# Running product: partial products summed in PSUM by TensorE, normalisation in four-step pieces

## The reference

```
mag = sqrt(a_re^2 + a_im^2);  scale = min(mag, 0.999) / (mag + 1e-6)
a_n = a * scale                                  # complex, per token and dimension
S_re, S_im = a_re_n*S_re - a_im_n*S_im + k (x) v, a_re_n*S_im + a_im_n*S_re
y[t] = q[t] . S_re
```

## Time and profile before

| | us |
|---|---|
| median of 3 runs | 813.38 (813.21 to 814.14) |
| profiled execution, its own time | 813.1 |
| its span | 811.3 |
| PE busy in the span | 674.3 (83%) |
| DVE busy | 655.7 (81%) |
| ACT busy | 480.1 (59%) |

### The profile page before, as it was taken

One profiled execution on the slowest core, in us unless ns is written; L12 is line 12 of the kernel. 1 busy time (PEld: TensorE's weight loads), 2 busy tenths in 40 slices (PEclk: granted clock), 3 DMA queues, 4 the chain that ended last, 5 costly groups with the idle time before them and its releaser, 6 DMA issues.

```text
span 811.3 us, 17899 instructions
## 1 busy us (share of the span) xinstructions
PE 674.3 (83%) x6792; PEld 630.3 (78%) x6792; DVE 655.7 (81%) x1241; ACT 480.1 (59%) x673; POOL 213.5 (26%) x183
## 2 busy tenths in 40 slices
PE   0634342089999999938999999999999999999997
PEld 0413231088888888928999999999999989999997
DVE  7998999989999999966868667756898687676572
ACT  7688898567766666453656555545644544554541
POOL 3200000011111111013343456632344332233422
PEclk9765655589999999969999999999999999999999
DMA  7221311018833333455765665667665755665640
GB/s 190 60 71 44 88 44 29 0 51 146 173 118 107 116 95 109 138 105 192 246 226 181 222 207 192 223 197 243 209 200 186 257 187 197 223 225 188 233 151 30
DMA packets 78342, 123.77 MB, mean 153 GB/s; under 512 B 12986, under 2 KB 60582, under 8 KB 78096
## 3 DMA queue, kind: packets, MB, share of 16 engines
q1 hardware_dynamic: 71120, 106.43, 43.2%
q0 software_dynamic: 7168, 16.64, 5.8%
HBM read 111.30 MB, written 13.75 MB: 154 GB/s over the span
## 4 chain that ended last, share of the span: by engine, by line
PE 46%; DVE 6%; DMA 2%; issue 1%; ACT 1%; POOL 0%; POOLq 0%; SPq 0%; DVEq 0%
PE banks L1281 20%; PE banks L1345 14%; PE banks L1328 8%; PE banks L1256 2%; DVE w_lo L899 2%; PE banks L1266 1%; DMA raw<-w1b 1%; DMA raw<-w1a 1%; DVE mix_spot L1544 1%; DVE mix_hT_lo L1643 1%; PE banks L1263 1%; DVE w_lo L905 1%; ACT w_hi L889 0%; DMA xbuf<-mix_y,to_scatter 0%; DVE mix_y L1667 0%
## 5 line engine op out<-in xcount | busy, mean ns | idle before, releaser
L1281 PE MATMUL banks<-mix_xT_hi,w_hi 128*128 128x240 f32 x576 | 159.8, 277 | 0.6 <-DVE mix_xT_lo L1652 0.6
L1281 PE MATMUL banks<-mix_xT_lo,w_hi 128*128 128x240 f32 x576 | 159.2, 276 | 0.0
L1281 PE MATMUL banks<-mix_xT_hi,w_lo 128*128 128x240 f32 x576 | 158.0, 274 | 0.0
L709 PE MATMUL banks<-sq,ident 128*128 128x288 f32 x104 | 49.7, 662 | 81.4 <-ACT sq L626 81.4
L1382 ACT ACTIVATE mix_hT_hi<-banks 128x480 fp32r<-128x480 f32 x96 | 54.8, 572 | 105.6 <-PE banks L1281 103.2
L1281 PEld LDWEIGHTS banks<-mix_xT_hi,w_hi 128*128 128x128 f32 x576 | 108.9, 189 | 0.9 <-issue 0.8
L1281 PEld LDWEIGHTS banks<-mix_xT_hi,w_lo 128*128 128x128 f32 x576 | 109.4, 190 | 0.0
L1281 PEld LDWEIGHTS banks<-mix_xT_lo,w_hi 128*128 128x128 f32 x576 | 109.2, 190 | 0.0
L709 PEld LDWEIGHTS banks<-sq,ident 128*128 128x128 f32 x104 | 32.7, 325 | 97.2 <-ACT sq L626 62.8
L1643 DVE SCALAR_TENSOR_TENSOR mix_hT_lo<-banks,mix_hT_hi 128x480 fp32r<-128x480 f32 x96 | 62.7, 653 | 55.7 <-ACT mix_hT_hi L1382 53.6
L1345 PE MATMUL banks<-w_hi,mix_hT_hi 128*128 128x384 f32 (+1 forms) x256 | 89.8, 351 | 1.5 <-DVE mix_hT_lo L1643 1.5
(11 more groups left out here) (236 smaller groups left out, 1696.9 us busy)
## 6 DMA issues: line engine op xcount, KB each, us to landing
raw<-w1b SPq DMA_DIRECT2D x16, 1536.0 KB, 7.8
raw<-w2b SPq DMA_DIRECT2D x16, 1536.0 KB, 6.7
raw<-w1a SPq DMA_DIRECT2D x8, 1536.0 KB
raw<-w2a SPq DMA_DIRECT2D x8, 1536.0 KB, 7.8
ring<-a SPq DMA_DIRECT2D x9, 864.0 KB, 4.9
qk<-q SPq DMA_DIRECT2D x48, 96.0 KB, 2.3
qk<-k SPq DMA_DIRECT2D x48, 96.0 KB, 2.3
vt<-v SPq DMA_DIRECT2D x24, 192.0 KB, 2.5
```

What stands on the lines that cost most here:

```text
L709: last = pe.matmul(banks[:, c, 0:STEP * PSEG].rearrange("p (t s) -> p t s", t=STEP), ident[:, :], sq[:, c * STEP:(c + 1) * STEP, j, :], st ...
L1281: last = pe.matmul(pU[g % TURNS][:, n * N:(n + 1) * N], w1p[m][:, b, c, f * P:(f + 1) * P], xT[s][:, c, 0:N], start=(c == 0 and (s, m) == ...
```

## The change

The sum of a step's partial products moves from VectorE to TensorE, and the running product lives in PSUM. `prod` for a half holds four blocks of 36: P_re*a_re, P_re*a_im, P_im*a_re, P_im*a_im. Three matmuls with a 128x128 identity, or with a negated identity, add them into a slot of 72 columns of a PSUM bank: 72 columns (start of the sum), 36 and 36. VectorE's next product reads the slot directly. Six steps (`BLOCK`) fill a bank; each half has a bank of its own and a second one in turn, so four banks are used. ScalarE copies out blocks of six steps (`spread_out(b)`), both planes and both halves in one copy of 864 elements.

The negated plane and all negations go; the ring has two planes and five groups, and its slot is free once its last product is formed. The squares' sums use banks 4 to 7 for odd and even groups, in matmuls of 216 columns that TensorE issues one at a time between the steps' matmuls (`squares_at`), three groups ahead. The normalisation's four instructions work on four steps each (288 and 576 elements), twelve instructions for a group of twelve steps, and VectorE issues one after most steps and two after a group's last (`parts_at`).

```diff
-    STEP, SPAN, RING = 4, 12, 4
+    STEP, SPAN, RING, BLOCK = 4, 12, 5, 6
...
+        def place_of(t):
+            return t // BLOCK % 2 * 2, t % BLOCK * SLOT
...
                 if g >= RING:
-                    sp.wait_ge(spread, g - RING + 1)
                     for c in range(2):
-                        sp.wait_ge(added[c], starts[g - RING + 1])
+                        sp.wait_ge(multiplied[c], starts[g - RING + 1] - 1)
...
+            def add(t, c):
+                first, col = place_of(t)
+                into = bank[first + c][:, col:col + SLOT]
...
+                if t % BLOCK == 0 and t >= 2 * BLOCK:
+                    pe.wait_ge(spread, t // BLOCK - 1)
+                pe.wait_ge(multiplied[c], t)
+                pe.matmul(into.rearrange("p (j s) -> p j s", j=2), ident[:, :], prod[:, c, RE], start=True, stop=False,
+                          skip_group_check=True)
+                pe.matmul(into[:, IM * HS:(IM + 1) * HS], ident[:, :], prod[:, c, IM, RE], start=False, stop=False,
+                          skip_group_check=True)
+                pe.matmul(into[:, RE * HS:(RE + 1) * HS], negated[:, :], prod[:, c, IM, IM], start=False, stop=True,
+                          skip_group_check=True).then_inc(added[c], 1)
...
+            def squares_at(g, n):
+                if g == 1:
+                    return {3: (3, (0, 1, 2)), 4: (3, (3, 4, 5)), 5: (3, (6, 7)), 6: (4, (0, 1)), 7: (4, (2, 3))}.get(n)
+                if g == 2 and n < 2:
+                    return 4, (2 * n + 4, 2 * n + 5)
+                if n >= 4 and g + 3 < GROUPS and n - 4 < count_of(g + 3):
+                    return g + 3, (n - 4,)
...
+            for t in range(T):
+                g = group_of[t]
+                if t == starts[4]:
+                    embed_turned()
+                for c in range(2):
+                    add(t, c)
+                piece = squares_at(g, t - starts[g])
+                if piece:
+                    sum_squares(*piece)
...
             def step(t):
-                if t == starts[group_of[t]] or t == 1:
-                    dve.wait_ge(negated, group_of[t] + 1)
+                if t == 1 or t % STEP == 0:
+                    dve.wait_ge(scaled, t // STEP + 1)
+                first, col = place_of(t - 1)
+                g = group_of[t]
                 for c in range(2):
-                    if t > 1:
-                        dve.wait_ge(added[c], t - 1)
-                    dve.tensor_tensor(prod[:, c], here(t - 1, IM, 2, c).unsqueeze(2).to_broadcast([P, 2, 2, HS]),
-                                      crossed(t, c), ALU.mult).then_inc(multiplied[c], 1)
-                for c in range(2):
-                    dve.wait_ge(multiplied[c], t)
-                    dve.tensor_tensor(here(t, IM, 2, c), prod[:, c, 0], prod[:, c, 1], ALU.add).then_inc(added[c], 1)
+                    dve.wait_ge(added[c], t)
+                    dve.tensor_tensor(prod[:, c],
+                                      bank[first + c][:, col:col + SLOT].rearrange("p (i s) -> p i s", i=2
+                                                                                  ).unsqueeze(2).to_broadcast([P, 2, 2, HS]),
+                                      ring[:, g % RING, t - starts[g], :, c * HS:(c + 1) * HS
+                                           ].unsqueeze(1).to_broadcast([P, 2, 2, HS]), ALU.mult).then_inc(multiplied[c], 1)
...
+            def parts_at(g, n):
+                if g == 0 or g + 1 == GROUPS:
+                    return 0
+                if g == 1:
+                    return 2 if n >= 2 else 0
+                if g == 2:
+                    return (0, 0, 0, 1, 1, 1, 1, 1, 1, 2, 2, 2)[n]
+                return (0, 1, 1, 1, 1, 1, 1, 1, 1, 1, 1, 2)[n]
```

More of the change, by code:

```diff
@@ L497, in running_products @@
     GROUPS = len(sizes)
-    assert sum(sizes) == T and all(s % STEP == 0 for s in sizes)
+    BLOCKS = -(-T // BLOCK)
+    assert sum(sizes) == T and all(s % STEP == 0 for s in sizes) and starts[2] == 2 * BLOCK and SPAN == 2 * BLOCK
     EARLY = 3
     group_of = [g for g, s in enumerate(sizes) for _ in range(s)]
-    IM, RE, NEG = 0, 1, 2
+    RE, IM = 0, 1
     HS = PSEG // 2
+    SLOT = 2 * HS
+    EMB = BLOCK * PSEG
+    ROUTE = EMB + KC * E
     with ExitStack() as ctx:
@@ L645, in inverses, with spread_out @@
                 act.activation(flat(recip, g), flat(recip, g), ACT.Exp, scale=-1.0).then_inc(exped, 1)
[L647 to L652, removed]
-                for c in range(2):
[L654 to L662, removed]
-                    for c in range(2):
[L664 to L668, removed]
+            def spread_out(b):
+                low, high = b * BLOCK, min(b * BLOCK + BLOCK, T)
+                first, _ = place_of(low)
+                for c in range(2):
+                    act.wait_ge(added[c], high)
+                if high < T:
+                    for c in range(2):
+                        act.wait_ge(multiplied[c], high)
+                else:
+                    act.wait_ge(ended, 2)
+                act.copy(A[:, :, 0:PSEG, low:high].rearrange("p j (c s) t -> p j c s t", c=2),
+                         banks[:, first:first + 2, 0:(high - low) * SLOT].rearrange(
+                             "p c (t j s) -> p j c s t", j=2, s=HS)).then_inc(spread, 1)
             act.preload_act_table_set("sqrt_and_others")
@@ L691, in _ @@
                     act.preload_act_table_set("natural_log_exp_and_others")
[L692 to L694 removed]
                     inverses(g + 2)
[L696 to L698 removed]
+                spread_out(2 * g - 2)
+            spread_out(BLOCKS - 1)
         @block.tensor
         def _(pe):
[L702 to L722 removed]
@@ new lines, in sum_squares @@
+            def sum_squares(g, pieces):
+                first = 4 + g % 2 * 2
+                for n in pieces:
+                    if n == 0:
+                        pe.wait_ge(squared, g + 1)
+                        pe.wait_ge(rooted, g - 1)
+                        if g == 9:
+                            pe.wait_ge(emb_copied, 1)
+                    low, j = n // 2 * (BLOCK // 2), n % 2
+                    high = min(low + BLOCK // 2, sizes[g])
+                    last = pe.matmul(bank[first + low // BLOCK][:, low % BLOCK * PSEG:(low % BLOCK + high - low) * PSEG],
+                                     ident[:, :], sq[:, g % 2, low:high, j, :], start=(j == 0), stop=(j == 1))
+                    if n == count_of(g) - 1:
+                        last.then_inc(summed, 1)
@@ L738, in clip @@
[L738 to L747 removed]
+            refined_at = {-1: 0}
@@ L808, in _ @@
             scale(0)
[L809 to L823 removed]
+            for t in range(1, starts[1]):
+                step(t)
```

209 lines of the change are left out of this document (125 added, 84 removed).

## The result

The changed kernel takes 1043.01 us (median of 4 runs, 1042.10 to 1044.16) against 813.76 us (813.21 to 814.57): a ratio of 1.2817, with a 95% interval of 1.2795 to 1.2839. The prediction was 800.3 us, in a range of 791 to 861. It had the wrong sign and the time is outside the range.

A forecast was written before the change was run, and what follows sets the result against it. VectorE was taken to bound the kernel's first stage, to about 163 us. The stage's sums end at 148.5 instead of 161.5 us, plus 0.2 for a longer end: -12.8 from 813.1 gives 800.3 us, range 791 to 861.

The forecast's parts named there:

- a step now needs six matmuls: TensorE, running product: six matmuls with 128x128 weights a step, 0.66 us at the full clock, 1.28 at the half.
- the clock rises in the second group and stays: TensorE's granted clock in the running product's stage goes to full in group two and remains; chance 0.50, 800.3 us.
- Rival A: Running product's stage: the half clock stays and TensorE binds, 18.5 us a group, 858.7 us in all; chance 0.36.
- the queue never empties, so it will rise: TensorE at the half clock: 1.28 us of work against a loop of 1.25 keeps it busy, so the clock rises.
- the rest of the forecast: Running product's stage with six matmuls a step at the full clock: it ends at 148.5 us against 161.5.
- the eight groups to step 120: Running product's stage at the full clock: a group of 12 steps takes 12.3 us in place of 13.5.
- the loop: Round trip of a half's step between VectorE and TensorE: 0.91 us at the full clock, 1.25 at the half.
- the three matmuls: TensorE's part of a half's round trip: 0.52 us at the full clock, 0.86 at the half.
- the last one, from which the forecast took 0.06 off: Last matmul of a half's three on TensorE: 36 columns instead of 113 make it 0.06 us shorter.
- the end of the stage and its handing over: Last product's copy out of PSUM ahead of ScalarE's last copy: 0.2 us longer.
- The product from PSUM: VectorE's product reading the PSUM slot: nothing extra charged, at worst 0.06 us a step, 8 us in all.
- rival C: Running product's stage: matmuls do not wait for weights, the loop is 0.65 us, VectorE binds, 786 us; chance 0.04.

The follow-up runs named there:

- experiment 2: The changed kernel with the running product's matmul calls widened by zeros to 108 and 116 columns, same sums: 884.31 us, ratio 1.0896.
- experiment 7: The changed kernel with fp32r products, squares and identities (one record a call), calls widened up to 292 columns, GpSimd's fill later: 825.35 us, ratio 1.0155.
- experiment 3: The changed kernel with the step's products and both identities in fp32r, one record a call, squares left at fp32: 886.41 us in a single execution.
- experiment 1: The kernel before with series of extra matmuls of 36 to 128 columns queued on TensorE after its last squares; whole time not compared.
- experiment 5: The changed kernel with GpSimd's fill of A's gap starting at step 24 instead of step 12: 1042.08 us.
- experiment 6: The changed kernel widened to 108 and 116 columns, with only the first of three matmul calls per half (four records a step): 819.11 us, ratio 1.0069.
- experiment 8: The kernel before with the clip of the normalisation factor moved from VectorE to GpSimd from group 3 on: 824.85 us, ratio 1.0147.

## Why the prediction was wrong, step by step

**The step that failed first was "a step now needs six matmuls".** It needs twelve. The trace of before had it: the burst of squares is x12 in the earlier trace rows, and the code issues six calls for a group there. I read the burst's length and not its count, and so took a squares' call for one record too. Its price is settled by experiments 2 and 7, both at the full clock: from twelve records to six (with the squares from two to one, and without the fill's 5 us) is 884.3 to 825.4, 59 us. At the half clock the same term weighs more: after against experiment 3 is 1043.0 to 886.4, 157 us, of which 4.6 are the fill's, and 127 steps x 6 x 0.213 is 162.

**The second is "the clock rises in the second group and stays".** Rival A had this right, with a chance of 0.36. The argument "the queue never empties, so it will rise" is refuted by experiment 1: 36 columns back to back stayed at 0.50. The doubt in rival A's own words, that the array streams columns for little of the time, was the right one. Its price is after against experiment 2: 159 us. Put right in the count of records alone, rival A's own sum comes out near: 858.7 + 127 x 1.28 + 70 x 0.36 = 1046.5, against 1043.0, in which 4.6 us are the fill's and not in that sum.

**The third is the rest of the forecast**, and experiment 7 shows it, since it has six records and the full clock: 827.9 in its profiled execution (2.6 above its median) against 800.3. Its last sum ends at 168.4 us instead of 148.5. Of these 19.9 us, 4.8 lie before step 12: 1.7 of them are a later first product, behind the making of the fp32r identities and the clearing of `prod`, and 1.3 are VectorE's instructions for the embeddings between steps 11 and 12, which the kernel before has there too and the forecast left out. Another 3.4 lie in the next group, which starts with a wait of TensorE for ScalarE's first copy out of PSUM and has the clock at 0.50 from 36.3 to 39.7 us; 10.4 in the eight groups to step 120 (13.6 each for 12.3), and 1.4 at the end.

```profile
35.77 0.40 PE L731 MATMUL banks<-prod,ident_r 128*128 128x292 f32 x1 [2.53 <-ACT A L678]
```

In the loop, VectorE follows TensorE after 0.04 us as forecast. TensorE follows VectorE after 0.05 us in 24 of the 33 cases from 51 to 160 us in which it stood idle, and after 0.15 in 9 (106.10 to 106.25 in experiment 7's rows). The 0.12 us that the loop is longer than forecast lie in the three matmuls, which take 0.64 us and not 0.52. About 0.07 of it is the last one, from which the forecast took 0.06 off because it moves only 36 columns. It takes 0.28 us with 256 columns (106.58 in experiment 7's rows), and the changed kernel, in its stretch at the full clock, takes 0.39 for two records 0.11 apart, so 0.28 with 36 columns as well:

```profile
37.44 0.39 PE L727 MATMUL banks<-prod,negated_ident 128*128 128x36 f32 x2
```

From the start of the last matmul to the start of the product it is 0.32 us in both. The rest is the first matmul of 292 columns (0.24 to the next one's start, 0.20 in the row that the forecast used).

The other 7.7 us lie behind the stage. The same ten microseconds in before and in experiment 7 (before has entered the attention stage 7 us earlier, so they are not the same work):

```profile
180.00:190.00 10.00, 10.00 (x188) 9.06 (x191) 9.71 (x13) 5.59 (x13) 2.55 (x2) 1.00 0.61 121
```

```profile
180.00:190.00 10.00, 10.00 (x109) 8.78 (x108) 5.04 (x6) 2.50 (x7) 1.19 (x1) 0.50 0.01 2
```

where DMA moves 121 and 2 GB/s too. In before the clock is at 0.50 for the first 4 us of the attention stage, in experiment 7 from 176.3 to 189.9 us. I had charged 0.2 us for the end of the stage and its handing over; which part the clock has in the 7.7 us was not tested.

**What held.** The product from PSUM takes 306 ns against 298 from SBUF: nothing extra. The pitch of a matmul behind a 128x128 weight load is 0.213 and 0.11 us down to 36 columns, so rival C (columns set the pace) is out. Pieces lie in VectorE's wait and are hidden. ScalarE's copy from PSUM takes 0.88 us for 864 elements, and in the changed kernel no wait of TensorE is put down to it. It is not always in time, though: at step 12 TensorE waits 1.0 us for it in experiment 5 and 2.5 us in experiment 7 (where VectorE's embeddings cover all but about 0.8). The later stages are 3 us longer in the changed kernel.

**What is not settled.** The series of experiment 1 have no pauses, and what pauses between such matmuls do was not measured by itself. The clock's fall at 126 us in experiment 6 comes 4 us after the squares end; why it falls was not tested by itself. Nor was a version with the same sums in fewer fp32 calls.

## What to carry to other kernels

Count records, not calls: divide the count of a line in the profile by the calls in the code before multiplying anything with a pitch. A matmul record in fp32 or fp32r with a full stationary matrix cost 0.11 or 0.21 us here even when it moved only 36 columns, so an identity matmul is a dear adder for 36 columns, and a chain of them that waits for VectorE had to beat VectorE's two sums, 0.29 us a step. And when TensorE's clock is part of a forecast, look for a row whose matmuls move as few columns as yours; in these runs a full queue was no evidence for it.

## What the runs showed of the hardware that was not expected

- The clock does not follow TensorE's busy share alone. With every stretch of experiment 1 busy throughout, it was 0.50 in the series of 36 columns, rose in those of 96 and 128, and kept in those of 72 the level that it had. The changed kernel stayed at 0.50 for 340 us of full work.
- fp32 calls are two records with two weight loads; fp32r and bf16 calls are one. In bf16, 120 matmuls of 36 columns took 3.16 us, 0.026 us each, weight loads included, against 0.112 in fp32 at the same clock. The Trainium skill (TensorE: Matmul & The Clock Gate, Weight-path perf modes) says that fast weight loads apply to 128 weights whose type is not fp32. The bf16 row agrees; the fp32r records, 0.11 us apart, do not show a faster load.
- VectorE slows down beside GpSimd, and by how much depends on the instruction: a TENSOR_SCALAR of 384 elements took 4.99 us beside a fill (0.407 alone), casts of 128 elements 3.8 and 3.9 us beside GpSimd's fills at the start of experiment 7, products of two SBUF operands 350 ns in the mean for 298 in experiment 8. The products of experiment 5 beside the same fill (from 81.2 us), which have one operand in PSUM, took 0.31 us as without it. The Trainium skill (GPSIMD Engine Reference, Specifications) says that GpSimd shares its SBUF interfaces with VectorE and contends with instructions of two SBUF inputs or in a two-port mode. The products of experiments 8 and 5 agree with it; in which mode the TENSOR_SCALAR and the casts ran, no row shows.
